# Two banks for the first up products, visits two products later, weights ahead of an alpha load, and block 2's low half behind an item's scores

## What is computed

```python
for t in range(S):                                  # attention, S = 768
    state = alpha[:, :, t, :, None] * state + np.einsum('bhd,bhe->bhde', k[:, :, t], v[:, :, t])
    y[:, :, t] = np.einsum('bhd,bhde->bhe', q[:, :, t], state)
x = y.transpose(0, 2, 1, 3).reshape(3072, 384)
h = x @ w_in;  x = (h * (1.0 / (1.0 + np.exp(-1.702 * h)))) @ w_out        # layer 1, 2048 hidden units
h = x @ w_in2; x = (h - np.tanh(h)) @ w_out2                               # layer 2
```

## Time and profile before

| | |
|---|---|
| median of 3 runs | 975.09 us |
| lowest and highest | 972.94 and 975.53 us |
| the profiled execution, device time | 973.15 us |
| its span | 971.4 us |
| TensorE, granted clock | 0.999 |
| TensorE busy | 949.3 us, 98% of the span |
| VectorE busy | 548.8 us, 57% |
| ScalarE busy | 334.6 us, 34% |
| GpSimd busy | 282.9 us, 29% |
| DMA | 58.87 MB, mean 61 GB/s |

### The profile page before, as it was taken

One profiled execution on the slowest core, in us unless ns is written; L12 is line 12 of the kernel. 1 busy time (PEld: TensorE's weight loads), 2 busy tenths in 40 slices (PEclk: granted clock), 3 DMA queues, 4 the chain that ended last, 5 costly groups with the idle time before them and its releaser, 6 DMA issues.

```text
span 971.4 us, 22253 instructions
## 1 busy us (share of the span) xinstructions
PE 949.3 (98%) x9354; PEld 820.3 (84%) x9354; DVE 548.8 (57%) x1348; ACT 334.6 (34%) x683; POOL 282.9 (29%) x314
## 2 busy tenths in 40 slices
PE   5899999999999999999999999999999999999998
PEld 4789999999999978888888888888888888888886
DVE  7879997877888877775221224334334333343332
ACT  1452333332332332323234554333333333332332
POOL 2666565646656554443002541000000000000000
PEclk9999999999999999999999999999999999999999
DMA  7944232423323322421204322020020010200001
GB/s 155 258 85 91 51 83 53 110 54 80 89 53 91 91 55 46 105 52 18 60 15 139 98 82 74 0 65 1 1 66 1 30 35 1 65 1 1 33 0 33
DMA packets 136229, 58.87 MB, mean 61 GB/s; under 512 B 114368, under 2 KB 131520, under 8 KB 136128
## 3 DMA queue, kind: packets, MB, share of 16 engines
q1 hardware_dynamic: 133488, 55.39, 22.9%
q10 hardware_dynamic: 2640, 2.05, 0.7%
HBM read 43.26 MB, written 13.96 MB: 59 GB/s over the span
## 4 chain that ended last, share of the span: by engine, by line
PE 92%; DVE 3%; DMA 2%; SPq 1%; POOL 1%; issue 1%; ACT 0%; DVEq 0%; POOLq 0%; ACTq 0%
PE pX L785 38%; PE pZ L809 27%; PE pX L809 14%; PE pX L649 2%; PE pZ L744 2%; PE pZ L677 2%; PE pZ L635 1%; PE pZ L687 1%; DMA k<-k_t 1%; PE pX L780 1%; PE pX L663 1%; PE pZ L735 1%; DVE scores L1093 1%; SPq L323 1%; DVE w_lo L1099 1%
## 5 line engine op out<-in xcount | busy, mean ns | idle before, releaser
L785 PE MATMUL pX<-x_hi,w_hi 128*128 128x512 f32 (+2 forms) x624 | 227.7, 365 | 0.7 <-ACT g L941 0.7
L785 PE MATMUL pX<-x_lo,w_hi 128*128 128x512 f32 (+2 forms) x624 | 227.3, 364 | 0.0
L785 PE MATMUL pX<-x_hi,w_lo 128*128 128x512 f32 (+2 forms) x624 | 227.3, 364 | 0.0
L1109 DVE TENSOR_TENSOR g_lo<-g,g_hi 128x512 fp32r<-128x512 f32 (+2 forms) x208 | 133.3, 641 | 155.1 <-ACT g_hi L950 154.9
L1207 DVE TENSOR_TENSOR g<-pX,sg 128x512 f32<-128x512 f32 x96 | 66.4, 691 | 177.6 <-ACT sg L943 177.6
L809 PE MATMUL pZ<-g_hi,w_hi 128*128 128x512 f32 (+2 forms) x414 | 150.9, 364 | 0.0
L809 PE MATMUL pZ<-g_lo,w_hi 128*128 128x512 f32 (+2 forms) x414 | 150.8, 364 | 0.0
L809 PE MATMUL pZ<-g_hi,w_lo 128*128 128x512 f32 (+2 forms) x414 | 150.8, 364 | 0.0
L950 ACT ACTIVATE g_hi<-g 128x512 fp32r<-128x512 f32 (+2 forms) x208 | 121.4, 584 | 78.1 <-DVE g L1207 74.5
L941 ACT ACTIVATE g<-pX 128x512 f32<-128x512 f32 (+3 forms) x144 | 65.8, 457 | 208.9 <-PE pX L785 175.7
L785 PEld LDWEIGHTS pX<-x_hi,w_hi 128*128 128x128 f32 x624 | 117.5, 188 | 17.9 <-ACT g L941 1.1
(11 more groups left out here) (100 smaller groups left out, 1133.6 us busy)
## 6 DMA issues: line engine op xcount, KB each, us to landing
v<-v_l SPq DMA_DIRECT2D x96, 48.0 KB, 2.6
x_raw<-hidden SPq DMA_DIRECT2D x6, 768.0 KB, 6.0
attn_out<-y SPq DMA_DIRECT2D x92, 48.0 KB, 1.8
out_t<-o SPq DMA_DIRECT2D x10, 384.0 KB, 3.5
alpha<-a_t SPq DMA_DIRECT2D x24, 128.0 KB, 2.9
r<-q_t SPq DMA_DIRECT2D x24, 128.0 KB, 3.0
k<-k_t SPq DMA_DIRECT2D x24, 128.0 KB, 3.0
w_raw<-w_in SPq DMA_DIRECT2D x16, 192.0 KB, 2.4
```

The lines of the kernel that those rows point to most:

```text
L785: last = nc.tensor.matmul(pH(N)[:, 0:w], win(wp, f, m), XS[T % 2][xp][:, m, 0:w], start=(n == 0), stop=(n == len(terms) - 1))
L1109: nc.vector.tensor_tensor(GL[:, columns(N)], g_raw(N), GH[:, columns(N)].bitcast(F32), ALU.subtract).then_inc(gl_done, 1)
```

## The change

- `pH(N)` gives `O0` in place of `H0` for N = 1 and N = 3, so that the first up products alternate between two banks. The waits on `g_done` follow: none before `up(1)`, one product less before `up(2)` to `up(4)`; `down(0)` to `down(3)` wait for four activations, since `down(0)` overwrites `O0`.
- Visits: items 3 to 7 stand behind `up(6)`, `up(10)`, `up(14)`, `up(18)`, `up(22)` in place of 4, 8, 12, 16, 20. Items from 8 on stay. `down(0)` now comes ahead of the visit of item 3 and waits for the states of items 0 and 1 itself.
- SP issues weight group 3 right behind group 2, ahead of the alpha load of unit 3.
- `plain_queries(U)` of units 2 to 5 stands at the step of the visit, behind that visit's copies, in place of one step ahead.
- `x_low(2)` on DVE moves from the end of step 29 to step 25, between `states(8)` and the rest of that step.

```diff
-    starts = ([0, 4, 8, 12, 16, 20, 25, 30] + ...
+    starts = ([0, 6, 10, 14, 18, 22, 25, 30] + ...
...
+XLOW_AT = {1: 9}
...
         def pH(N):
+            if N in (1, 3):
+                return O0
             return H0 if N < L1B * NF or N % 2 == 0 else H1
...
                 if U == 1:
                     load_w(sp, 2)
+                    load_w(sp, 3)
                 if U + 2 < UNITS:
                     load_alpha(U + 2)
-                if U == 1:
-                    load_w(sp, 3)
...
                 if N < L1N:
-                    if N:
-                        pe.wait_ge(g_done, N)
+                    if N > 1:
+                        pe.wait_ge(g_done, N if N > 4 else N - 1)
...
                 if T < PLAIN:
-                    pe.wait_ge(g_done, N + 1)
+                    pe.wait_ge(g_done, max(4, N + 1))
...
+                if N == 0:
+                    pe.wait_ge(state_step, states_before(LEAD))
...
-            queries_at = {VISIT_OF[j + 1] - 1: j // 2 + 1 for j in range(LEAD, ITEMS - 2, 2)}
+            queries_at = {VISIT_OF[j + 1] - (VISIT_OF[j + 1] >= L1P): j // 2 + 1 for j in range(LEAD, ITEMS - 2, 2)}
...
                         scores(j, low)
                         states(j)
+                        if XLOW_AT.get(T) == f:
+                            x_low(T + 1)
                         ahead(j, 0)
...
-                if f == x_at(T) and PLAIN <= T + 1 < ALLB:
+                if f == x_at(T) and T not in XLOW_AT and PLAIN <= T + 1 < ALLB:
                     x_low(T + 1)
```

More of the change, by code:

```diff
@@ L128, in visits @@
 def visits():
-    starts = ([0, 4, 8, 12, 16, 20, 25, 30] + [33 + 3 * n for n in range(5)] + [49 + 3 * n for n in range(5)]
+    starts = ([0, 6, 10, 14, 18, 22, 25, 30] + [33 + 3 * n for n in range(5)] + [49 + 3 * n for n in range(5)]
               + [64 + 2 * n for n in range(29)])
@@ L940, in _ @@
                 if T < L1B:
-                    nc.scalar.activation(g_raw(N), H0[:, 0:width(T)], ACT.Gelu_apprx_sigmoid).then_inc(g_done, 1)
+                    nc.scalar.activation(g_raw(N), pH(N)[:, 0:width(T)], ACT.Gelu_apprx_sigmoid).then_inc(g_done, 1)
                 else:
```

## The result

| | kernel before | changed kernel |
|---|---|---|
| median of 20 runs each | 973.51 us | 976.32 us |
| lowest and highest | 971.66 and 977.50 us | 973.37 and 980.36 us |
| profiled execution, its span | 971.4 us | 976.3 us |
| profiled execution, granted clock | 0.999 | 0.996 |

The ratio of changed to before is 1.0023, with a 95% interval of 1.0012 to 1.0033: the change costs about 2.2 us, where 1.8 us of gain were predicted. The interval doesn't reach 1, so the change does cost time, though less than the 0.3% that the prediction called no change. 976.32 is above the top of the predicted range.

The account below looks back on a forecast made before the run. TensorE was nearly always busy, DVE nearly as full. Gains of 2.7 and 2.1 us made 4.8, cut by DVE to 1.6; plus 0.4, less 0.2 for alpha, 1.8: 973.3 us from 975.09, range 970.9 to 975.7.

Parts of the forecast that it names:

- Two banks: First up products: without their waits, four more products are done before item 3's visit, which stays at 34.93; gain 2.7 us.
- Queries: Visit of item 5: with the queries' copy behind it, the wait for transposed keys goes; gain 2.1 us.
- Weights ahead of alpha: SP's load queue: alpha lands at 44.9 behind group 3, 4.1 us per group; cost at visit 5 0 to 0.2 us.
- the prediction's own chain: Alpha to visit 5: products up to 2.8 us, scores of item 4 from 47.6, done 4.02 us later at 51.6.
- third rival: Loads ahead of visit 5: weights hold alpha until 50.0, past break-even at 46.7, giving 978.4 us; chance 0.09.
- the visits until item 8: Items 4 to 8: scores are ready in time, so item 8's visit starts at 74.99 in place of 79.83.
- 4.8 us: TensorE's lead at item 8's visit, the sum of 2.7 and 2.1, before DVE limits it at item 10.
- Collision with POOL: DVE's key product, 1.07 us beside POOL: POOL is done by then, which may give back 0.4 us.
- `x_low`: Block 2's low half on DVE, step 25: DVE idles 1.5 us waiting for ACT's high half, queued work behind it.

Follow-up runs that it names:

- e9: The changed kernel once more, nothing edited, timed and profiled anew: 976.13 us against 973.72 for the kernel before, ratio 1.0027.
- e10: The kernel before with only the queries' copies of units 2 to 5 moved to the visit's step, behind its copies: 972.93 us, ratio 0.9994.
- e2: The kernel before with only weight group 3 issued ahead of unit 3's alpha load: 974.14 us against 974.17, ratio 1.0007.
- e3: The changed kernel with the up product of step 14 made five times, filling TensorE's idle time ahead of visit 5: 976.71 us, ratio 1.0034.
- e8: The changed kernel with up products repeated (step 14 five times, 30 and 33 three times) to fill idle times ahead of visits 5, 9, 10: 976.90 us.
- e1: The changed kernel with weight group 3 issued behind unit 3's alpha load again: 974.60 us against 974.17 for the kernel before, ratio 1.0006.
- e7: e6 with all twelve alpha steps in one row at the visit of item 7 in place of two parts: 972.56 us, ratio 0.9982.
- e6: The changed kernel with e5's order of loads in place of the early group 3, and `x_low` at its old place: 973.44 us, ratio 0.9991.
- e4: e1 with `x_low` of block 2 also back at its old place, the end of step 29: 973.98 us, ratio 1.0001.
- e5: The kernel before with weight group 3 split, first half right behind alpha, second behind unit 3's keys: 972.17 us against 974.11, ratio 0.9983.
- e12: e7 with `x_low(2)` on DVE at step 27 in place of 29: 972.33 us against 973.72 for the kernel before, ratio 0.9982.

## Why the prediction was wrong

**Two banks: right as a step.** Eight products stand ahead of the visit of item 3, and it starts at 35.19 (34.93 before). The lead of TensorE is 2.7 us less what the gap in the first down product takes, which the prediction had at nothing: 0.26 us in this trace, 1.2 in e9, where the gap is 1.28 and visit 3 stands at 36.14.

**Queries: right as a step.** e10 shows visit 8 sooner by 2.4 us, 0.3 of it there at the start, against 2.1 predicted.

**Weights ahead of alpha: the term of the sum that was mis-sized.** I had alpha at 44.9 and "0 to 0.2 us"; it landed at 47.38 and 47.76 (46.94 in e2). The slip is in the price of a group: 4.1 us was how much longer a load took that was issued right behind one group. The trace after has the last weights in only at 46.6. Taken as the prediction took it, with 2.7 us for alpha behind the queue, two groups took (47.4 - 2.7 - 34.0) / 2, about 5.3 us each, an estimate. With alpha at 47.4 the prediction's own chain (products 2.8, now 3.2 with POOL's product in the way, then 4.02 to the visit) gives 54.6; measured 54.55. The break-even of its third rival, 46.7, was passed by 0.7, so this rival came true in kind, with alpha at 47.4 and not its 50.0; it had a chance of 0.09. The Trainium skill's rule that the prediction quoted (DMA: Bandwidth & Descriptors, Queues, rings and completion order) holds for each DMA engine by itself. The prediction read it as "alpha can't land before group 3 has", and that is stronger than the traces: the first half of alpha is in at 39.24 + 6.8 = 46.0, 0.5 us ahead of the last weights, the second half at 47.4 behind them. What they do show is alpha 4.1 to 4.9 us late behind one group more, in the two traces and in e2.

**The clock: missing.** An idle time was priced at its own length. In the changed kernel's trace visit 5's 2.71 us cost 2.5 us more at 0.50 clock. e3 and e8, in which TensorE works through it, show that it is the idle time that does it; e9 shows that an execution can be spared.

**DVE: the step that failed most.** The prediction said of the visits until item 8 that "the scores that it needs are ready", and moved DVE with TensorE from 55 us on. But in the earlier trace rows DVE waits 2.58 us for the keys of unit 3 at 52.64, on POOL and so on their load. With the weights where they were (e1) that doesn't move when TensorE comes sooner; with the weights early it is alpha that holds DVE. e1 has scores 5 at 55.88, where the prediction's chain needs them near 53.6; its scores 7 start at 71.99 in place of my 70.2, and those of item 8 at 82.58 in place of 79.4. So already at the scores of item 8 nothing of the 4.8 us was left, and visit 10, which I put at 96.5, came at 99.14.

**Collision with POOL: seen with the wrong sign.** I gave DVE 0.4 us back because POOL would be done. The 0.4 at the key product came (0.68 in place of 1.07 in e9), but the same shift put POOL's products between DVE's short steps of alpha, which cost 2.9 us in the changed kernel (1.27, 1.19, 0.70 and 0.59 in place of 0.18, 0.19, 0.17 and 0.30). e7 takes the steps out of the way, and its scores of item 8 start 2.2 us sooner than e6's.

**`x_low`: wrong.** ACT's part was right: `x_hi` starts 9.51 us behind visit 8, predicted 9.43. But DVE came late itself, so there was no 1.5 us of idle time, and e4 differs from e1 by 0.6 us, too little to be told from nothing by their intervals.

**The sum.** At the full clock the change costs 1.3 us by the counted runs; e1 puts 1.7 of the 2.2 to 2.8 us on the weights, with the clock in it. What stays open is how the cost divides between the clock and DVE, because e3 and e8 hold the clock at visit 5 but pay 1.7 to 1.8 us for other things. Why the clock falls in some executions and not in others at the same place was not tested.

## What to carry to other kernels

When the fuller of two coupled engines is 90% busy, follow its chain, with what it waits for, before counting a lead of the other: here 4.8 us of TensorE's lead were gone at DVE's scores of item 8 (e1), while e5, which gave DVE its keys sooner and TensorE no lead, is the fastest kernel together with e7 and e12. Price a load behind others by when the queue is drained of all bytes ahead of it, not by the extra latency of one load behind one group. And an idle time of TensorE can cost nearly twice its length, through the clock, as visit 5 did here.

## What the runs showed of the hardware

- **Clock.** After TensorE idled 2.71 us (changed), 4.09 (e1, at visit 10), 2.62 (e3, at visit 10), 2.37 (e6, at visit 9) or 1.15 us (e5, at visit 3), the granted clock was 0.50 in the stretch behind it; after 2.03 us (before), 1.06 (e9) and, at visit 10, 2.64 (changed) and 2.65 us (e9) it stayed at 1.00. The same length of idle time gave either, and before the 1.15 us of e5 there are three waits of 0.37 us that the kernel before has too, without the fall.
- **DVE and POOL.** Steps of 0.18 and 0.19 us took 1.27 and 1.29 when they started within 0.1 us behind the start of a POOL product of 1.3 us (changed, e6), and ended with it; a POOL product of 1.27 us took 3.79 when it fell into a row of DVE's low halves (e7). The Trainium skill gives a reason (SBUF — State Buffer, SBUF: two separate sides): the two engines share a port pair as an exclusive lock, held for a whole instruction by the one that starts first. The steps agree with it. That POOL stays out for a whole row of DVE's instructions, and that it makes a difference in which gap its product begins, is what e6 and e7 add.
- **Loads.** 128 KB of alpha took 2.7 to 3.0 us with nothing large ahead of it, 6.8 behind group 3 issued 3.1 us earlier (5.6 in e9, 5.9 in e2), with the DMA engines at 295 GB/s from 33 to 46 us.
